# Three-layer block on one core: gate reciprocals and second-half mixes moved to other steps, part of the mixes on ScalarE

## The reference

```python
def _moe_ref(x, mu_k, mu_r, w_k, w_v, w_r) -> np.ndarray:
    B, S, D = x.shape
    x_prev = np.concatenate([np.zeros((B, 1, D), dtype=np.float32), x[:, :-1, :]], axis=1)
    xk = mu_k * x + (1.0 - mu_k) * x_prev
    xr = mu_r * x + (1.0 - mu_r) * x_prev
    k = np.maximum(xk @ w_k, 0.0)
    v = k * k @ w_v
    r = 1.0 / (1.0 + np.exp(-(xr @ w_r)))
    return (r * v).astype(np.float32)
```

## Time and profile before

| | |
|---|---|
| median of 3 executions | 616.51 us (616.0 to 616.89) |
| profiled execution | 616.65 us |
| span of its instructions | 614.8 us |
| mean granted TensorE clock | 0.975 |
| busy: PE, DVE, ACT, POOL | 561.2, 385.3, 233.0, 240.8 us |
| longest parts of the chain that ended last | PE L473, L475, L474: 46% together; DVE gate L986 4%; POOL `c_prob` L1210 3% |

### The profile page before, as it was taken

One profiled execution on the slowest core, in us unless ns is written; L12 is line 12 of the kernel. 1 busy time (PEld: TensorE's weight loads), 2 busy tenths in 40 slices (PEclk: granted clock), 3 DMA queues, 4 the chain that ended last, 5 costly groups with the idle time before them and its releaser, 6 DMA issues.

```text
span 614.8 us, 12183 instructions
## 1 busy us (share of the span) xinstructions
PE 561.2 (91%) x5008; PEld 490.9 (80%) x5008; DVE 385.3 (63%) x766; ACT 233.0 (38%) x583; POOL 240.8 (39%) x287
## 2 busy tenths in 40 slices
PE   6578879999989998999989998999998998999987
PEld 4467879999757987999855998899965798999654
DVE  4877998681458689464257689657145869361451
ACT  2473313322564322422366331342256341222464
POOL 4625964631245344341134254243024553331231
PEclk9689879999999999999999999999999999899999
DMA  8961202111002120221000320100000200000002
GB/s 268 398 225 41 70 0 70 32 39 30 2 2 78 40 69 2 69 70 30 1 2 10 109 56 14 30 2 1 2 1 1 78 2 2 1 1 1 1 1 78
DMA packets 8934, 29.61 MB, mean 48 GB/s; under 512 B 1200, under 2 KB 1200, under 8 KB 8880
## 3 DMA queue, kind: packets, MB, share of 16 engines
q1 hardware_dynamic: 6256, 24.12, 12.0%
q10 hardware_dynamic: 2624, 4.72, 2.4%
HBM read 24.12 MB, written 4.72 MB: 47 GB/s over the span
## 4 chain that ended last, share of the span: by engine, by line
PE 63%; DVE 18%; ACT 6%; POOL 6%; issue 3%; DMA 2%; SPq 1%; POOLq 0%; DVEq 0%
PE MM L473 16%; PE MM L475 15%; PE MM L474 15%; DVE gate_r L986 4%; POOL c_prob L1210 3%; PE SC L437 3%; PE OA L462 3%; PE MM L567 3%; PE OA L616 2%; DMA raw_wr_lo<-in_w_r 2%; ACT c_prob L763 2%; DVE mix L939 2%; PE TR L449 2%; DVE ring L966 2%; DVE c_negmax L1044 2%
## 5 line engine op out<-in xcount | busy, mean ns | idle before, releaser
L1182 POOL TENSOR_TENSOR k_lo<-ring,k_hi 128x288 fp32r<-128x288 f32 x64 | 57.2, 897 | 99.5 <-ACT k_hi L744 99.2
L1210 POOL TENSOR_SCALAR c_prob<-c_prob,c_inv,gates 128x512 f32<-128x512 f32 (+3 forms) x64 | 41.9, 663 | 127.8 <-DVE c_inv L1054 127.8
L473 PE MATMUL MM<-k_hi,wv_hi 128*128 128x288 f32 x256 | 78.1, 305 | 8.7 <-POOL k_lo L1182 4.9
L473 PE MATMUL MM<-act_hi,wk_hi 128*128 128x288 f32 x256 | 78.0, 305 | 2.5 <-POOL wk_lo L1219 2.5
L474 PE MATMUL MM<-k_lo,wv_hi 128*128 128x288 f32 x256 | 76.6, 299 | 0.0
L475 PE MATMUL MM<-k_hi,wv_lo 128*128 128x288 f32 x256 | 76.4, 298 | 0.0
L474 PE MATMUL MM<-act_lo,wk_hi 128*128 128x288 f32 x256 | 76.0, 297 | 0.0
L475 PE MATMUL MM<-act_hi,wk_lo 128*128 128x288 f32 x256 | 75.9, 297 | 0.0
L966 DVE TENSOR_TENSOR ring<-ring 128x288 f32<-128x288 f32 x64 | 45.2, 717 | 47.0 <-ACT ring L757 46.5
L986 DVE RECIPROCAL gate_r<-gate_r 128x288 f32<-128x288 f32 x32 | 62.5, 1953 | 1.1
L473 PEld LDWEIGHTS MM<-k_hi,wv_hi 128*128 128x128 f32 x256 | 49.1, 192 | 11.3 <-POOL k_lo L1182 6.7
(11 more groups left out here) (159 smaller groups left out, 1377.6 us busy)
## 6 DMA issues: line engine op xcount, KB each, us to landing
qkT<-in_qk SPq DMA_DIRECT2D x16, 591.5 KB, 3.9
vn<-in_v SPq DMA_DIRECT2D x16, 432.0 KB, 3.7
out_x<-c_prob ACTq DMA_DIRECT2D x16, 224.0 KB, 2.4
raw_wk_lo<-in_w_k SPq DMA_DIRECT2D x4, 512.0 KB, 16.4
raw_wv_lo<-in_w_v SPq DMA_DIRECT2D x4, 512.0 KB, 18.7
raw_wr_lo<-in_w_r SPq DMA_DIRECT2D x2, 512.0 KB, 14.3
out_x<-c_prob ACTq DMA_DIRECT2D x4, 256.0 KB, 2.9
raw_cv_lo<-in_c_v SPq DMA_DIRECT2D x1, 520.0 KB, 16.5
```

Source lines behind the costliest of these rows:

```text
L473: nc.tensor.matmul(dst, w2[0], x2[0], start=first, stop=False)
L1182: nc.gpsimd.tensor_tensor(lo, ring[:, ITEM[u] % RING, :], hi.bitcast(fp32), ALU.subtract)\
L1210: nc.gpsimd.tensor_scalar(prob_tile(u), prob_tile(u), c_inv[:, u:u + 1], gate, ALU.mult, ALU.mult).then_inc(c_prob, 1)
```

## The change

The order of the units and the matmuls is the same in both kernels. Three things differ.

- `PIECE`: the second half's mixes stand at steps 0, 1, 4, 5 (k, t 0 to 3) and 6, 8, 9, 11 (r, t 0 to 3).
- In these eight, ScalarE makes the product with mu (`act_scale`) and the rounding (`act_mix_hi`, one step later); DVE keeps `scalar_tensor_tensor`. The eight mixes of the first half stay on DVE. A new semaphore `mix_scaled` counts ScalarE's products.
- `R_AT`: gates stand at steps 7, 10, 12, 13 and 20, 22, 24, 26.

```diff
--- before.py
+++ after.py
@@ -125,10 +125,17 @@
     PIECE = [(-2, "r", 0, t) for t in range(KT)] + [(-1, "k", 0, t) for t in range(KT)]
-    PIECE += [(KT, "k", 1, 0), (KT + 2, "r", 1, 0)]
-    PIECE += [(KT + FT - 3 + t, "r", 1, t) for t in range(1, KT)]
-    PIECE += [(KT + FT + 1 + t, "k", 1, t) for t in range(1, KT)]
+    PIECE += [(step, "k", 1, t) for t, step in enumerate((0, 1, 4, 5))]
+    PIECE += [(step, "r", 1, t) for t, step in enumerate((6, 8, 9, 11))]
+    R_AT = {7: (0, 0), 10: (0, 1), 12: (0, 2), 13: (0, 3), 20: (1, 0), 22: (1, 1), 24: (1, 2), 26: (1, 3)}
     PIECES = len(PIECE)
+
+    MIX_STEPS = [2 if x[2] == 0 else 1 for x in PIECE]
+    HALF_1 = [j for j in range(PIECES) if PIECE[j][2] == 1]
+
+    def mixes_before(b, j):
+
+        return b * sum(MIX_STEPS) + sum(MIX_STEPS[0:j])
...
@@ -838,6 +846,34 @@
+        def act_scale(act_, b, j):
+
+            _, what, half, t = PIECE[j]
+            m = 0 if what == "k" else 1
+            if j == HALF_1[0]:
+
+                act_.wait_ge(x_ready, (b + 1) * PAIRS * 2)
+            before = max([x for x in range(j) if PIECE[x][3] == t], default=-1)
+            act_.wait_ge(mix_lo, b * PIECES + before + 2)
+            nc.scalar.activation(mix[:, t * HALF:(t + 1) * HALF], xT[:, t, 1 + half * HALF:1 + (half + 1) * HALF],
+                                 ACT.Copy, scale=mus[:, m, t:t + 1]).then_inc(mix_scaled, 1)
+
+        def act_mix_hi(act_, b, j):
+
+            _, what, half, t = PIECE[j]
+            if (what, t) == ("r", 0):
+
+                act_.wait_ge(mm_full, b * MMS + KT)
+            act_.wait_ge(mix_step, mixes_before(b, j + 1))
+            nc.scalar.activation(mix_target(j)[0], mix[:, t * HALF:(t + 1) * HALF], ACT.Copy).then_inc(mix_hi, 1)
+
@@ -848,6 +884,12 @@
                 act_item_hi(act_, b, i - 1)
                 if ahead:
                     act_attention(act_, b + 1, i, EXP)
+                for j in HALF_1:
+                    if PIECE[j][0] == i - 1:
+                        act_mix_hi(act_, b, j)
+                for j in HALF_1:
+                    if PIECE[j][0] == i:
+                        act_scale(act_, b, j)
             act_experts(act_, b)
...
@@ -931,20 +966,21 @@
-            before = max([x for x in range(j) if PIECE[x][3] == t], default=-1)
-            dve.wait_ge(mix_lo, b * PIECES + before + 2)
-            nc.vector.tensor_scalar(slot, xT[:, t, 1 + half * HALF:1 + (half + 1) * HALF],
-                                    mus[:, m, t:t + 1], None, ALU.mult).then_inc(mix_step, 1)
-            dve.wait_ge(mix_step, (b * PIECES + j) * 2 + 1)
+            if half == 0:
...
+            else:
+                dve.wait_ge(mix_scaled, b * len(HALF_1) + HALF_1.index(j) + 1)
             nc.vector.scalar_tensor_tensor(
                 out=slot, in0=xT[:, t, half * HALF:(half + 1) * HALF],
                 scalar=one_less[:, m, t:t + 1], in1=slot, op0=ALU.mult, op1=ALU.add)\
                 .then_inc(mix_step, 1)
...
+            if half == 0:
+                dve.wait_ge(mix_step, mixes_before(b, j) + 2)
+                nc.vector.tensor_copy(mix_target(j)[0], slot).then_inc(mix_hi, 1)
...
@@ -974,9 +1010,9 @@
         def dve_r(dve, b, u):
 
-            if u + 1 >= B_UNITS or UNIT[u + 1][1] != "v":
+            if u not in R_AT:
                 return
-            half, _, n = UNIT[u + 1]
+            half, n = R_AT[u]
```

More of the change, by code:

```diff
@@ L311, in build @@
         x_ready = sem("x_ready")
+        mix_scaled = sem("mix_scaled")
         mix_step = sem("mix_step")
@@ L839, in act_experts, with mix_target @@
                                cp[n % 3][0:m, 0:DM]).then_inc(out_done[n % 3], 16)
+        def mix_target(j):
+            _, what, half, t = PIECE[j]
+            if what == "r":
+                return [a[:, t * HALF:(t + 1) * HALF] for a in xr]
+            return [a[:, t * S + half * HALF:t * S + (half + 1) * HALF] for a in act]
+        def act_scale(act_, b, j):
[8 more added lines that the diff above has]
+        def act_mix_hi(act_, b, j):
+            _, what, half, t = PIECE[j]
+            if (what, t) == ("r", 0):
+                act_.wait_ge(mm_full, b * MMS + KT)
+            act_.wait_ge(mix_step, mixes_before(b, j + 1))
+            nc.scalar.activation(mix_target(j)[0], mix[:, t * HALF:(t + 1) * HALF], ACT.Copy).then_inc(mix_hi, 1)
         GATE_STEPS = 18
@@ L913, in dve_attention @@
                     dve_step(dve, bb, p, o)
[L915 to L920, removed]
         def dve_mix(dve, b, j):
@@ L932, in dve_mix @@
                 dve.wait_ge(x_ready, (b + 1) * PAIRS * 2)
-            before = max([x for x in range(j) if PIECE[x][3] == t], default=-1)
-            dve.wait_ge(mix_lo, b * PIECES + before + 2)
-            nc.vector.tensor_scalar(slot, xT[:, t, 1 + half * HALF:1 + (half + 1) * HALF],
-                                    mus[:, m, t:t + 1], None, ALU.mult).then_inc(mix_step, 1)
-            dve.wait_ge(mix_step, (b * PIECES + j) * 2 + 1)
+            if half == 0:
+                before = max([x for x in range(j) if PIECE[x][3] == t], default=-1)
+                dve.wait_ge(mix_lo, b * PIECES + before + 2)
+                nc.vector.tensor_scalar(slot, xT[:, t, 1 + half * HALF:1 + (half + 1) * HALF],
+                                        mus[:, m, t:t + 1], None, ALU.mult).then_inc(mix_step, 1)
+                dve.wait_ge(mix_step, mixes_before(b, j) + 1)
+            else:
+                dve.wait_ge(mix_scaled, b * len(HALF_1) + HALF_1.index(j) + 1)
             nc.vector.scalar_tensor_tensor(
```

## The result

| | before | after |
|---|---|---|
| median of the runs on one chip | 616.25 us (613.75 to 618.51, 6 runs) | 622.88 us (620.96 to 627.16, 6 runs) |
| profiled execution, span | 616.65, 614.8 us | 622.86, 621.1 us |
| mean granted clock | 0.975 | 0.970 |

A forecast was written before the change was run, and what follows sets the result against it. TensorE was taken to bound the kernel, so other engines' changes only open or close its waits and move the clock. Terms -8.4 + 5.9 + 6.2 + 3.4 = +7.1 us on 616.5 gave 623.6 us, range 611.5 to 631.

The forecast's parts named there:

- gated products and their half clock: Steps 12 to 15: TensorE's waits for gated products in batches 1 to 3 and a half clock go, -8.4 us.
- first halves: Step 12 in all batches: the last low half of k comes later, +5.9 us together.
- second halves: All four gates now precede the last square, so the last low half of k comes later, +6.2 us together.
- half clock: Longer waits bring up to four stretches of 3.4 us at half clock, 6.8 us; half taken, +3.4 us.
- First half, batches 1 and 2: Step 12: 3.5 us more DVE work against 2.3 of slack, plus ScalarE's delay; 1.6 us each, 0 to 2.0.
- The lower bound: First half, batches 1 and 2: 0 if DVE reaches step 10 in time and its gate delays scores by 1.0 us.
- First half, batch 3: Same DVE excess against 2.4 us of idle time, no attention to widen steps: 1.4 us, at most 2.2.
- The ScalarE blocking: Waiting for a mix blocks ReLUs behind it on ScalarE; priced at nothing except in batch 3, inside its bound.
- Second half, batches 1 and 2: Four gates (9.5 us) before the last square, 7.0 us hidden by idle time: 1.3 us each, 0.8 to 2.5.
- Second half, batch 0: Squares wait behind POOL's 2.58 us `co_lo`, then a gate: last low half 2.0 to 3.0 us late, 2.7 taken.
- the port relief: Rival: products and casts leaving DVE free its port with POOL, every wait takes its lower end; 611.1 us, chance 0.27.
- Everything late: Rival: all waits at their upper ends, batch 0's pair of waits doubling; +16.0 us, 632.5 us, chance 0.15.

The follow-up runs named there:

- the share alone: Kernel before with only product and cast of the second-half mixes moved to ScalarE, mixes and gates at their old steps: 602.02 us, ratio 0.9780.
- the first experiment: Changed kernel with the first-half gates back at steps 11 to 14: 608.93 us, ratio 0.9904.
- the k mixes first: Kernel before with ScalarE making the second-half mixes' product and cast, k mixes at steps 0 to 3, r at 6, 11 to 13: 599.47 us, ratio 0.9758.

## Why the prediction was right, and where it was not

The forecast of 623.6 us was 0.7 above the measured 622.88, with the mechanism named: no wait for gated products, longer waits for the last `k_lo` in both halves, half clock behind some of them. The four terms:

| term | predicted | measured |
|---|---|---|
| gated products and their half clock | -8.4 | -8.2 (6.7 of waits, a stretch at 1.5) |
| first halves | +5.9 | +6.2 |
| second halves | +6.2 | +4.4 |
| half clock | +3.4 | +4.5 (three stretches at 1.5) |
| sum | +7.1 | +6.9 |

The medians differ by 6.6, the profiled executions by 6.2. Of the 0.7 that the sum is over the latter, 0.4 is the lead that the run of after had before its second stage began. The small error of the forecast is in part luck. The terms' errors cancel, 1.8 too much for the second halves against 1.1 too little for the clock and 0.3 for the first halves; and the runs of the changed kernel lie between 620.96 and 627.16 us with mean granted clocks from 0.975 to 0.956, so that three stretches in the profiled run are one outcome of several.

- *Gated products.* Right as to what went, wrong as to whom to thank. I gave the gain to the mixes and the two gates that leave steps 12 to 15. With all gates back it stays, and the share alone already has all of it in batches 1 to 3 (and 1.1 us of a new wait in batch 0). Beside the share the gate moves bought nothing.
- *First half, batches 1 and 2.* I took 1.6 us between 0 and 2.0; 1.96 came, the upper end. The sum over DVE's time (3.5 us more, 2.3 of slack) had the size right and treated all additions alike. One gate did it: the added work of the whole stretch used up the slack, and the gate of step 10, next to the scores that stand ahead of the last square, came through whole. It needs both: with that gate behind the square the wait is 0.48, with that gate in place but the mixes at their old steps it is 1.65. The lower bound named this tail, but only as a delay of 1.0, since it supposed 1.2 us of waiting for the scores that no longer existed.
- *First half, batch 3.* Taken 1.4, bound 2.2; 2.80 of waits against 0.88 is +1.9. The ScalarE blocking, which I had let in for this batch only, showed as 0.38 us of waiting for a bank. It takes the gate of step 7 as well: ScalarE's high half waits for the square behind that gate (next row), then two passes for mixes (0.45 and 0.52 us) come before the ReLU. With either the first half's gates or the mixes at their old steps the bank wait is gone.

```profile
511.30 0.45 ACT L752 ACTIVATE k_hi<-ring 128x288 fp32r<-128x288 f32 x1 [1.45 <-DVE ring L1002]
```

- *First half, batch 0.* Taken 1.3, between 0 and 3.6; the waits in its steps 2 to 12 sum to 6.6 where they were 6.2, +0.4. Its two stretches of half clock swapped their lengths.
- *Second half, batches 1 and 2.* Taken 1.3, bound 0.8 to 2.5; 0.59 came, below my lower end. I had DVE's idle time right as the cover (it fell from 7.5 + 1.2 to 2.0 us), and the walk through the tail right in kind. The lower end failed because it let nearly all of the scores' shift of 1.0 reach the high half: in batch 1 TensorE stands 5.3 us later than before at this place, the scores end 6.2 later (275.58), but the high half starts only 5.9 later (276.44), since before the exponential had waited 0.3 us for ScalarE, and now it follows the scores at once. Batch 3, which has no scores, has the same wait, 0.58. Moving the gate of step 26 behind the last square removed it in all three.
- *Second half, batch 0.* Taken 2.7; +2.63 came, from the two causes named, and each is needed.
- *Clock.* Priced at half of four stretches of 1.7. Three came, in batches 0, 1 and 2, at about 1.5 each.

Of the rivals, the port relief was not imaginary. The casts and products that leave DVE had been dear there: by rows, the 32 second-half ones of each took 17.5 us (31.2 - 13.7) and 17.0 us (14.3 + 13.1 - 10.4) before.

```profile
L947 DVE CAST xr_hi<-mix 128x288 fp32r<-128x288 f32 x32 | 13.1, 408 | 1.4
...
L973 DVE TENSOR_SCALAR mix<-xT,mus 128x288 f32<-128x288 f32 x32 | 13.7, 428 | 0.1
```

The first row is of the kernel before, the second of the share alone, where only the first-half ones are left: 13.7 us for products and 10.4 for casts. The second-half ones thus took 0.53 to 0.55 us each; with POOL idle a cast takes 0.31 and a product 0.30 to 0.37, so by this estimate 13 to 15 of the 34.5 us that left DVE were delay beside POOL. The squares that stay gained little, from 717 to 694 ns. The forecast was right to let the added gates outweigh it, and the point at which it said it would decide, DVE's square of step 10 starting when its ReLU ends, was missed by 0.8 us (ReLU done at 224.21, square at 225.04). Everything late stayed away: batch 0's pair of waits did not double (3.23 us before, 1.32 + 0.95 + 1.06 after), and the second halves stayed under its ends.

What stays open: how much of the share's 13.3 us is the port and how much is DVE's own time. The rows give the shares of DVE's busy time, but no run separates a DVE that is busy from one that is barred where TensorE waits.

## What to carry to other kernels

A long instruction that fills an engine's idle time is free only until the next piece of work with a due time: put the gate behind the last square, not ahead of what that square waits for, and the same 2.4 us cost nothing instead of 2.65 us of wait and a half clock. When a change has three parts, account each with and without the others; here one part made the gain and another, meant for the same wait, had nothing left to win. Where a wait needs two causes, either one taken away cures it.

## What was not expected of the hardware

- **The clock behind a wait.** Among the waits of batches 1 to 3 and of batch 0's second half, none of 1.66 us or less was followed by a half clock, and those of 1.80 us and more sometimes: 3.13 us yes and 3.14 no in one trace; 2.70 us yes in after and no in the first experiment. I found no feature that separates them, so such a stretch has a chance and a price, about 1.5 us. In batch 0's first half, where several waits stand close together, a stretch also began behind one of 1.29 us (the k mixes first). The Trainium skill, "TensorE: Matmul & The Clock Gate", section "Why this matters for your kernels", asks that TensorE be left no long idle gaps between bursts if the clock is to stay up. The traces agree in that these falls stand in or behind waits; a long gap alone did not decide it here, since 3.14 us brought none in one trace.
- **The start.** The half clock in the first stage of batch 0 was 17.1 us long in before and in after, 13.7 with the second-half gates back and 10.2 in the share alone; 1.1 us of that kernel's profiled lead arose there. Single profiled runs should be compared stage by stage for that reason.
- **DVE beside POOL.** In the timeline of after the gate's first instruction takes 0.91 us while a POOL subtraction runs, 0.30 in the experiment that moved it to a free moment; `scalar_tensor_tensor` takes 1.08 there and 0.46 to 0.52 with POOL idle or about to end. Beside POOL's 2.59 us instruction the gate's first one took 2.47 us (new gate steps alone). The reciprocal took 1.95 to 1.96 us in all 32 cases of after, with POOL at work beside each of them for part of its time. So the new place of an instruction can change its own price by a factor of two to eight, and that of another not at all.
